# Two attention bursts moved ahead of one group of weight products on TensorE, and two SBUF spacers taken out or shortened

## The reference

```python
def _attn_ref(r, k, v, w, u):
    state = np.zeros((B, H, D, D))
    for t in range(S):
        cur = np.einsum('bhd,bhe->bhde', u[None] * kt, vt)
        y[:, :, t] = np.einsum('bhd,bhde->bhe', rt, state + cur)
        state = w[None, :, :, None] * state + np.einsum('bhd,bhe->bhde', kt, vt)
    return y

def _moe_ref(x, w1, w2, w3, w_out):       # 384 -> 1024 -> 1024 -> 384
    a = x @ w1
    b = x @ w2
    h = a * b @ w3
    return h @ w_out

def _moe2_ref(x, w_in, w_out):            # 384 -> 2048 -> 384
    h = x @ w_in
    g = h * np.cos(h)
    return g @ w_out
```

## Time and profile before

| | us |
|---|---|
| median of 3 runs | 792.42 |
| lowest and highest | 791.97 and 792.66 |
| the profiled execution: its time | 792.66 |
| the profiled execution: its span (first to last instruction) | 791.2 |

### The profile page before, as it was taken

The page is one execution under the profiler, slowest core; times in us unless marked ns, Lnnn a source line. Parts: engine busy times, 40 slices in busy tenths (PEclk is TensorE's granted clock), DMA queues, the critical chain, the costliest instruction groups (busy, mean ns, idle before and its releaser), DMA issues.

```text
span 791.2 us, 15799 instructions
## 1 busy us (share of the span) xinstructions
PE 784.6 (99%) x6500; PEld 677.2 (86%) x6500; DVE 429.4 (54%) x639; ACT 376.4 (48%) x647; POOL 345.8 (44%) x279
## 2 busy tenths in 40 slices
PE   8999999999999999999999999999999999999998
PEld 6999999888999888998888888888888888888886
DVE  7998655543644433123289555546555554554553
ACT  4634222222222222224367667656665765665664
POOL 2646766556566553111234335334333432433432
PEclk9999999999999999999999999999999999999999
DMA  8775445342344320202221010000001001001001
GB/s 335 267 244 149 114 145 152 91 137 85 105 139 144 89 88 22 80 0 73 68 80 41 2 41 0 1 8 33 1 1 40 1 1 40 1 1 39 2 1 40
DMA packets 47595, 57.32 MB, mean 72 GB/s; under 512 B 21794, under 2 KB 34211, under 8 KB 47523
## 3 DMA queue, kind: packets, MB, share of 16 engines
q1 hardware_dynamic: 34898, 45.83, 17.9%
q10 hardware_dynamic: 12624, 10.49, 4.3%
HBM read 46.86 MB, written 9.44 MB: 71 GB/s over the span
## 4 chain that ended last, share of the span: by engine, by line
PE 96%; DVE 3%; issue 1%; ACT 0%; POOL 0%; DVEq 0%; POOLq 0%
PE p_h L1164 25%; PE p_acc L1164 13%; PE p_a L1164 13%; PE p_b L1164 13%; PE p_out L1385 8%; PE p_out L1381 8%; PE p_out L1382 8%; PE p_s L1188 2%; PE p_y L1200 1%; PE p_y L1204 1%; PE p_acc L1313 1%; PE p_kv L1192 1%; DVE w3t_l L982 1%; PE p_b L1320 0%; PE p_acc L1299 0%
## 5 line engine op out<-in xcount | busy, mean ns | idle before, releaser
L626 POOL TENSOR_TENSOR g_l<-g,g_h 128x512 fp32r<-128x512 f32 x96 | 149.9, 1561 | 241.6 <-ACT g_h L814 241.6
L1113 DVE TENSOR_TENSOR g<-angle,p_h 128x512 f32<-128x512 f32 x96 | 65.8, 686 | 109.1 <-ACT angle L823 109.1
L490 POOL TENSOR_TENSOR g_l<-g,g_h 128x384 fp32r<-128x384 f32 (+1 forms) x56 | 70.2, 1253 | 121.0 <-ACT g_h L663 121.0
L1381 PE MATMUL p_out<-g_h,wq_l 128*128 128x512 f32 x288 | 112.1, 389 | 0.0
L1164 PE MATMUL p_h<-y_l,wi_h 128*128 128x512 f32 x288 | 112.1, 389 | 0.0
L1164 PE MATMUL p_h<-y_h,wi_h 128*128 128x512 f32 x288 | 112.1, 389 | 0.0
L1164 PE MATMUL p_h<-y_h,wi_l 128*128 128x512 f32 x288 | 112.1, 389 | 0.0
L1382 PE MATMUL p_out<-g_h,wq_h 128*128 128x512 f32 x288 | 112.0, 389 | 0.0
L814 ACT CAST g_h<-g 128x512 fp32r<-128x512 f32 x96 | 59.7, 621 | 67.5 <-PE p_out L1385 42.3
L658 ACT COPY g<-p_a 128x384 f32<-128x384 f32 (+1 forms) x56 | 29.4, 526 | 119.1 <-PE p_a L1164 117.5
L819 ACT ACTIVATE angle<-angle 128x512 f32<-128x512 f32 x96 | 60.6, 631 | 49.6 <-DVE angle L1123 49.6
(11 more groups left out here) (118 smaller groups left out, 1642.2 us busy)
## 6 DMA issues: line engine op xcount, KB each, us to landing
krT_raw<-in_kr_dims SPq DMA_DIRECT2D x24, 512.0 KB, 4.1
kr_raw<-in_kr_tokens SPq DMA_DIRECT2D x24, 384.0 KB, 4.7
v_raw<-in_v_tokens SPq DMA_DIRECT2D x24, 192.0 KB, 4.8
x_raw<-y_transposed SPq DMA_DIRECT2D x24, 192.0 KB, 2.5
out<-out_sb SPq DMA_DIRECT2D x17, 256.0 KB, 2.0
stage_b<-in_moe_w_in SPq DMA_DIRECT2D x8, 384.0 KB, 3.1
stage_b<-in_moe_w_out SPq DMA_DIRECT2D x8, 384.0 KB, 3.0
y_transposed<-yT ACTq DMA_DIRECT2D x24, 96.0 KB, 2.6
```

The lines of the kernel that those rows point to most:

```text
L490: nc.gpsimd.tensor_tensor(g1_l[:, n % 2, cols], g1[:, n % 2, cols], g1_h[:, n % 2, cols].bitcast(F32), ALU.subtract).then_inc(s_gl, 1)
L626: nc.gpsimd.tensor_tensor(g2_l[:, par, :], g2[:, par, :], g2_h[:, par, :].bitcast(F32), ALU.subtract).then_inc(s_g2l, 1)
L1113: nc.vector.tensor_tensor(g2[:, n % 2, :], angle[:, n % 2, :], p_h[n % 4][:, :], ALU.mult).then_inc(s_g2, 1)
L1381: mm(bank[t][:, :], wq_l[:, f, cols], g2_h[:, f % 2, :], start=f == 0, stop=False)
```

## The change

It does two things.

**The order on PE.** The bursts `burst(2, 1)` and `burst(3, 2)` come eight products earlier: right behind `w34_highs` of tiles 4 and 5, where they stood behind `w34_high_low`. `burst(1, 0)` stands there already. The instructions and their waits stay the same, and the lists of ACT, DVE, POOL and SP are the same, instruction for instruction.

**The layout of SBUF.** `to_lines` goes (32 bytes a partition), and `over_att` shrinks from 64 to 44 numbers, which is 64 bytes less after rounding up to 32. Every tile from `kr_raw` to `over_att` starts 32 bytes lower, and every tile from `w1_h` on 96 bytes lower. Before, `kr_raw` and `wi_h` start at byte 56576 of a partition, `w1_h` at 112128 and `x_raw` at 161280, all multiples of 256; now at 56544, 112032 and 161184, which are 32 past a multiple of 64. `wo_h`, `w3_raw`, `stage_more` and `y2` lie below and stay.

```diff
-    to_lines = sb("to_lines", [P, 8])
...
-    over_att = sb("over_att", [P, 64])
+    over_att = sb("over_att", [P, 44])
...
             for t in range(NF):
                 w34_highs(f, t)
-            if f == WHOLE + 1:
-                burst(1, 0)
+            if WHOLE < f <= WHOLE + HC:
+                burst(f - WHOLE, f - WHOLE - 1)
             if f == WHOLE:
                 pe.wait_ge(s_stl, NWO)
             for t in range(NF):
                 w34_high_low(f, t)
-            if WHOLE + 2 <= f <= WHOLE + HC:
-                burst(f - WHOLE, f - WHOLE - 1)
             pe.wait_ge(s_wtl, f - WHOLE + 1)
             for t in range(NF):
                 ins = w34_low_high(f, t)
```

## The result

| | before | changed | ratio, 95% interval |
|---|---|---|---|
| median, us | 792.26 | 799.64 | 1.0099, 1.0082 to 1.0116 |
| profiled execution: its time | 792.66 | 801.15 | |
| profiled execution: its span | 791.2 | 799.6 | |

The change costs 7.4 us. The profiled execution of the changed kernel lies 1.5 us above its median, so its span shows 8.4.

What follows compares the result with a forecast made beforehand. PE's instruction list was taken to bound the kernel. Waits of 1.14 + 0.02 us, less 0.97 given back, made +0.19, with layout at zero; on the median of 792.42 that gave 792.6 us, range 791.7 to 794.0.

Steps and rivals of the forecast that it cites:

- The reading of the bottleneck: Whole kernel: PE, busy 784.6 of 791.2 us, sets the end; only its waits or its products' pace can change it.
- each step: PE, tiles 4 to 6: burst(2, 1) starts at 31.73, tile 6 at 43.13, its second group at 44.54.
- The sum of +0.19 us: PE, both moved bursts: new waits of 1.14 + 0.02 us paid, 0.97 us of old losses given back.
- I take zero for PE, by that row: Layout's cost on PE's products: 0, since products on stage_a and stage_more both take 486 ns.
- The layout slows products by 1 ns each: Rival on PE's products behind the prologue: the layout slows each by 1 ns, giving 795.8 us; chance 0.08.
- The bounds of 0.5 and 1 ns: Layout's bound on about 3,240 products behind the prologue: 1.6 us at 0.5 ns each, 3.2 at 1 ns, either sign.
- 789.2: Rival on PE's products: the layout speeds each up by 1 ns, giving this time in us; chance 0.03.
- the spread of 0.4 us: Whole time: spread of the runs before, said to be allowed on each side of the range.
- The clock: Rival on PE: products get slower by a rest of PE; chance 0.04.
- zero for the transfers and for DVE's work: Prologue: the layout costs transfers and DVE's work nothing; a landing 0.9 us later might delay DVE's list 0 to 0.9.
- The prologue: Rival there: the layout delays transfers or DVE, lengthening the rT_sc wait; up to +0.9 us, 793.5; chance 0.17.

Runs made afterwards that it cites:

- the run with both at 256: Kernel before, with y2_h and y2_l of the odd groups of 512 tokens both 256 bytes past their place: 792.92 us (one run).
- the run with 32: Kernel before, with y2_h and y2_l of the odd groups of 512 tokens both 32 bytes past their place: 797.12 us (one run).

## Why the prediction was wrong

**The reading of the bottleneck was right.** PE's list sets the end (PE is busy for 99% of the span in both profiles), and only waits or slower products could change it.

**The order, right in each step.** The burst at 31.72, tile 6 at 43.10, its second group at 44.51 in the run with the order alone; the waits for `w3t_l` and `w_l` gone; a new one of 1.0 us. The sum of +0.19 us stands beside a measured ratio of 1.0003 (0.9995 to 1.0012), which is +0.2 us, with an interval from -0.4 to +1.0. That single times agree to 0.03 us is partly luck: it needs a DVE list that is as early as in the kernel before, and in other profiles the same `rT_sc` came up to 1.2 us later.

**The layout, wrong: "I take zero for PE, by that row."** This is the step that failed: the term for the layout on PE, put at 0, measured 7.3 us in the run with the layout alone. It rested on the earlier trace rows, where products on `stage_a` and on `stage_more` take 486 ns both. By distance this row is even a fair comparison: the weights `w_raw` start 128 past a multiple of 256, so `stage_a` is at 128 from them and `stage_more` at 0. What was wrong is to carry it over to other products. Those of the earlier trace rows are of whole float32 and follow each other every 323 ns, nearly twice the time of the split products of 384 columns, with a weight load of 190 ns beside each. They show no loss at 128; the split products do. That they have less room is a reason that was not tested. The row to read was in the same trace: the groups of w3 x w_out, at a distance of 128, take 1.41 us for eight products (0.176 each), while nine products of the same width in the first block, at 0, take 52.98 - 51.42 = 1.56 (0.173 each):

```profile
51.42 0.34 PE L1164 MATMUL p_a<-x_h,w_l 128*128 128x384 f32 x1
...
52.98 0.33 PE L1164 MATMUL p_b<-x_h,w_l 128*128 128x384 f32 x1
```

Those 3 ns were an effect of the distance, as the run with `wo_h` shifted shows.

**The rival was on the list, too small and with too little chance.** "The layout slows products by 1 ns each", chance 0.08, 795.8 us. Measured were 6 to 7 ns on 864 products and 1 to 2 on 576 of the others, not 1 ns on 3,240. The bounds of 0.5 and 1 ns came from no row; the range ended at 794.0, since the rival's price was left out of it. (Two small slips changed nothing: 792.6 - 3.2 is 789.4, not 789.2, and the spread of 0.4 us was added at the range's upper end only.) An unused tile whose only effect is where the tiles behind it start, in a kernel in which PE is busy for 99% of its time, deserved that the distances of all operand pairs be written down before and after. That table alone would have shown that one pair of four loses its distance of 0.

**The clock.** No run shows what the chance of 0.04 stands for, products that get slower by a rest of PE. In the changed kernel the granted clock is 1.000 as before, and behind the wait of 1.16 us the burst takes 34.21 - 32.20 = 2.01 us and the group after it 35.73 - 34.21 = 1.52, the lengths of the earlier trace rows.

**The layout outside PE.** The prediction took zero for the transfers and for DVE's work, and the whole time shows no cost of it: with every tile from `kr_raw` on 32 bytes lower the kernel took 792.26 us (one run), beside 792.35 of the kernel before.

**The prologue.** DVE's `rT_sc` of chunk 2 ended 0.5 us later than before in the profile of the changed kernel and 1.2 us later in that with `over_att` at 64, but not in that of the order alone, and 0.2 us later in that of the layout alone. The new addresses are not needed for it. In the run with both at 256, which has the old order and every tile of the prologue at its old place, the same instruction began at 31.69 instead of 30.94, and PE waited for it at two bursts, 0.33 and 0.87 us:

```profile
PE p_y L1201 <- DVE rT_sc L880: 1.2, 2, 0.9
```

So the prologue differs from execution to execution by itself. Whether the layout adds to that is open; the medians leave at most some tenths for it.

**Open:** why the distance counts. In the trace of the kernel before, the weight load of a product `y_l, wi_h` (0.19 us) starts at 450.84, together with the product ahead of it, `y_h, wi_l` (0.39 us). That loads and products get into each other's way at some distances is my guess; no run shows it. The values at single distances (0 and 256 free, 64 cheap, 32, 128 and 192 dear) follow no rule that I could find, and neither does the way in which the loss spreads to neighbours at distance 0.

## What to carry to other kernels

Write down, for each kind of product, how far its moving operand starts from its weights in a partition, modulo 256, and keep it at 0 for all of them, since one kind that is off slowed its neighbours too (by 2 to 7 ns in the run with 32); check it again after every edit of an allocation, also of tiles that nobody uses. If a change moves addresses and PE is the bottleneck, compare the mean duration of each product group first: the loss here, up to 7 ns a product, showed in no wait and no clock (1.000). And before an input's wait is taken out of cover, see how steady the producer's end is: the same burst waited 1.0 us in one profile and 2.3 in another.

## What the runs showed of the hardware

- Split products of 512 columns take 389 ns on the page in the second block when weights and moving operand of all kinds in the mix start a multiple of 256 bytes apart (256 itself was tried). With `p_h` off, its means are 394 to 396 at 32, 392 to 396 at 128, 395 to 396 at 192 and, with all kinds off, 388 to 394 at 64; `p_out` off at 192 has 393 to 398.
- Products at distance 0 in such a mix lose too: up to 2 ns in the changed kernel (`p_h` at 192), 2 to 7 ns in the run with 32.
- Products of 384 columns lose 3 ns at 192. Eight of them in the weight product take 1.41 us from start to start at 128, and 1.39 at 0 and at 224.
- Small products of 64 columns showed no loss at 64 (216 ns), and those of whole float32 none at 128 (486 ns, 323 from start to start).
- Where the pair starts made no difference: 0 and 224 past a multiple of 256 gave the same 389 ns.
